# Loading kv in 8 KB rows, and written-out orders for the first and last group of two chained feed-forward layers

## The reference, cut to what matters

```python
# q: 12288 x 128, kv: 384 x 32 x 128
kv_pool = kv.reshape(B, H//4, 4, W//4, 4, C).mean(axis=(2, 4))    # 96 x 8 cells of 4 x 4 pixels
k = v = kv_pool.reshape(B, -1, C) @ w_sr                          # 768 keys
a = softmax(q @ k.T / sqrt(C))                                    # sum gets + 1e-9
x = a @ v
h = x @ w_in1                                                     # 128 -> 2048
x = (max(h, 0) + alpha * min(h, 0)) @ w_out1                      # first layer
h = x @ w_in2                                                     # second layer
out = ((a0 + a1 h + a2 h^2 + a3 h^3) / (1 + |b0||h| + |b1| h^2 + 1e-6)) @ w_out2
```

## Time and profile before

| | |
|---|---|
| median of 3 runs | 1563.15 us (1561.4 to 1563.31) |
| the profiled execution | 1564.52 us; its span in the trace 1562.7 us |
| busy share of the span | TensorE 97%, VectorE 92%, ScalarE 90%, GpSimd 79% |
| load and pooling of kv | up to 36.4 us |
| attention | 36.4 to 322.4 us |
| first layer of group 0 alone | 322.4 to 363.5 us |
| both layers | 363.5 to 1504.6 us |
| second layer of group 23 alone, and the last store | 1504.6 to 1562.7 us |

### The profile page before, as it was taken

How to read it: one execution, slowest core, us unless ns; L and a number is a source line. 1 busy time by engine, 2 the same in 40 slices (tenths; PEclk the granted TensorE clock), 3 DMA queues, 4 the chain that set the end, 5 groups by cost and what they waited for, 6 DMA issues and landing times. The chain is left out here.

```text
span 1562.7 us, 28287 instructions
## 1 busy us (share of the span) xinstructions
PE 1509.7 (97%) x8269; PEld 1242.8 (80%) x8269; DVE 1432.4 (92%) x2257; ACT 1401.7 (90%) x2714; POOL 1237.9 (79%) x1352
## 2 busy tenths in 40 slices
PE   5999999979999999999999999999999999999986
PEld 5899999846788888888888888888888888888865
DVE  4788888727999999999999999999999999999997
ACT  1777777637999999999999999999999999999996
POOL 0444444405999999999999999999999999999998
PEclk9999999999999999999999999999999999999998
DMA  8110110000000000000000000000000000000000
GB/s 244 48 28 22 28 48 21 1 0 1 8 1 8 8 8 8 2 8 8 8 1 8 8 8 8 1 8 8 8 8 1 8 8 8 1 8 8 8 8 8
DMA packets 12330, 24.94 MB, mean 16 GB/s; under 512 B 1536, under 2 KB 1680, under 8 KB 11920
## 3 DMA queue, kind: packets, MB, share of 16 engines
q1 hardware_dynamic: 11424, 22.55, 4.8%
q10 hardware_dynamic: 752, 0.60, 0.1%
HBM read 16.85 MB, written 6.29 MB: 15 GB/s over the span
## 5 line engine op out<-in xcount | busy, mean ns | idle before, releaser
L270 POOL TENSOR_TENSOR cubic<-sq,lin_p 128x512 f32<-128x512 f32 x384 | 495.6, 1291 | 84.3 <-ACT sq L458 59.7
L261 POOL TENSOR_TENSOR rational<-newton,ratio 128x512 f32<-128x512 f32 x336 | 434.0, 1292 | 29.5 <-PE banks L1073 21.2
L1073 PEld LDWEIGHTS banks<-wout,rational 128*128 128x128 f32 x3072 | 399.8, 192 | 44.0 <-issue 11.0
L880 PE MATMUL banks<-x_hi,win_lo 128*128 128x512 f32 x768 | 387.1, 504 | 25.6 <-DVE ratio L747 13.5
L1073 PE MATMUL banks<-wout,rational 128*128 128x128 f32 x3072 | 402.7, 276 | 3.8 <-POOL rational L261 3.8
L882 PE MATMUL banks<-x_hi,win_hi 128*128 128x512 f32 x768 | 303.4, 395 | 0.0
L881 PE MATMUL banks<-x_lo,win_hi 128*128 128x512 f32 x768 | 302.9, 394 | 0.0
L476 ACT ACTIVATE lin_p<-banks,ab_raw 128x512 f32<-128x512 f32 x384 | 298.4, 777 | 1.0 <-PE banks L882 1.0
L730 DVE SCALAR_TENSOR_TENSOR banks<-sq,abs_b,banks 128x512 f32<-128x512 f32 x384 | 286.9, 747 | 2.9 <-ACT banks L468 2.5
L738 DVE SCALAR_TENSOR_TENSOR banks<-banks,ab_raw,cubic 128x512 f32<-128x512 f32 x384 | 288.3, 751 | 0.8 <-POOL cubic L270 0.8
L747 DVE SCALAR_TENSOR_TENSOR ratio<-banks,ab_raw,rcp 128x512 f32<-128x512 f32 x384 | 285.7, 744 | 1.8
(11 more groups left out here) (91 smaller groups left out, 2261.3 us busy)
## 6 DMA issues: line engine op xcount, KB each, us to landing
early<-in_kv_dram SPq DMA_DIRECT2D x24, 256.0 KB, 10.1
out_dram<-y_out SPq DMA_DIRECT2D x24, 256.0 KB, 2.0
neg_part<-in_q_dram SPq DMA_DIRECT2D x22, 256.0 KB, 2.7
early<-in_moe_w_in_dram SPq DMA_DIRECT2D x1, 1024.0 KB, 16.4
wout<-in_moe_w_in_dram SPq DMA_DIRECT2D x1, 1024.0 KB, 5.2
neg_part<-in_q_dram ACTq DMA_DIRECT2D x2, 256.0 KB, 9.3
early<-in_w_sr_dram ACTq DMA_DIRECT2D x1, 64.0 KB, 1.9
wout<-in_moe_w_out_dram SPq DMA_DIRECT2D x2, 0.5 KB, 12.6
```

The source lines that it names most:

```text
L261: nc.gpsimd.tensor_tensor(rational[:, m % 3, :], newton[:, m % 2, :], ratio[:, m % 2, :], ALU.mult).then_inc(s["rat_done"], 1)
L270: nc.gpsimd.tensor_tensor(cubic[:, m % 2, :], sq[:, m % 2, :], lin_p[:, m % 2, :], ALU.mult).then_inc(s["cubic_done"], 1)
L880: nc.tensor.matmul(dst, w[1], x[0], start=start, stop=False)
L1073: last = nc.tensor.matmul(banks[:, ACC2, t * P:(t + 1) * P], rational[:, m % 3, t * P:(t + 1) * P], wout2[:, c, :], start=(c == 0 and t == ...
```

## The change

1. **kv.** A partition now holds one image row (32 pixels) of each third of the image, and a chunk is one half of it: 16 pixels, 8 KB that lie together in memory. Five transfers of 1 MB and two of 512 KB take the place of 24 of 256 KB. A cell is thus spread over four partitions. A chunk has four units of 32 cells; in a unit four pixels lie side by side in a partition. TensorE sums over partitions and pixels at once, with a matrix of 128 x 32 with ones (`row_sums`, made by VectorE from the identity): four matmuls of 32 columns for a unit. For 14 of the 24 units (`BY_DVE_UNITS`) VectorE sums the four pixels first (512 elements to 128), and one matmul is left. The order of the keys changes, for k and v alike.
2. **Coefficients.** Their two broadcasts move from ACT's queue to SP's, behind w_out1, and the Abs of them to behind attention, ahead of the register loads.
3. **End of attention.** The split of w_out1 (`out1_hi`, `out1_lo`) moves into step 24 of attention, and hidden1 of group 0, block 0 into its last step.
4. **First group.** hidden1 has two banks, 0 and 1, in turn while n < 16, and waits for the block before last. The orders of all engines for the periods 0 and 1 are written out.
5. **Last group.** The periods from 24 on are written out for all engines, in an order of their own, and in group 23 VectorE makes five finals (2, 6, 10, 14, 15) in place of two. The loop bodies stay and run for p = 2 to 23.

```diff
 BY_DVE_FINAL, BY_DVE_RELU = (4, 12), (14,)
+LAST_DVE_FINAL = (2, 6, 10, 14, 15)
...
-    kv_rows = kv[0].rearrange("(hh r) (ww x) c -> hh ww r (x c)", r=POOL_SIDE, x=POOL_SIDE)
+    kv_rows = kv[0].rearrange("(k h) (n w) c -> k n h (w c)", h=P, n=2)
+    CELLS = P // POOL_SIDE
+    UNITS = P // CELLS
...
-        DVE_PIXELS, POOLED, VALUES = 2 * POOL_SIDE, (2, 3, 5, 6, 7, 2), (3, 6)
+        BY_DVE_UNITS = ((0, 1, 2), (0, 1), (0, 1), (0, 1, 2), (0, 1), (0, 2))
...
-        H1, ACC1, QV, H2, ACC2 = 0, 2, (3, 4), (5, 6, 1), 7
+        H1, ACC1, QV, H2, ACC2 = (0, 1), 2, (3, 4), (5, 6, 1), 7
...
+        def dve_finals(g):
+            return LAST_DVE_FINAL if g == GROUPS - 1 else BY_DVE_FINAL
...
+        def h1_bank(n):
+            return H1[n % 2 if n < BLOCKS else 0]
...
-            for c in range(CHUNKS):
-                for r in range(POOL_SIDE):
-                    sp.dma_start(kv_in[:, c, r * POOL_SIDE * P:(r + 1) * POOL_SIDE * P],
-                                 kv_rows[c * key_rows:(c + 1) * key_rows, :, r, :]).then_inc(s[f"ld_kv{c}{'aabb'[r]}"], 16)
+            for c in range(CHUNKS - 1):
+                sp.dma_start(kv_in[:, c, :], kv_rows[c // 2, c % 2]).then_inc(s[f"ld_kv{c}"], 16)
+            half = UNITS // 2 * POOL_SIDE * P
+            sp.dma_start(kv_in[:, CHUNKS - 1, 0:half], kv_rows[CHUNKS // 2 - 1, 1, :, 0:half]).then_inc(s[f"ld_kv{CHUNKS - 1}"], 16)
+            sp.dma_start(kv_in[:, CHUNKS - 1, half:], kv_rows[CHUNKS // 2 - 1, 1, :, half:]).then_inc(s["ld_kv_rest"], 16)
             sp.dma_start(raw_in[0], w_in1).then_inc(s["ld_in1"], 16)
             sp.dma_start(wout1[:], w_out1.rearrange("(b p) c -> p b c", p=P)).then_inc(s["ld_out1"], 16)
+            sp.dma_start(ab_raw[:, 0:4], coef_p.partition_broadcast(P)).then_inc(s["ld_ab"], 16)
+            sp.dma_start(ab_raw[:, 4:6], coef_q.partition_broadcast(P)).then_inc(s["ld_ab"], 16)
...
+                if g == GROUPS:
+                    out1_hi()
...
+            act.wait_ge(s["ld_ab"], 32)
+            nc.scalar.activation(abs_b[:], ab_raw[:, 4:6], ACT.Abs).then_inc(s["absb_col_done"], 1)
+            act.wait_ge(s["absb_col_done"], 1)
             scale_b0, scale_a3 = act.alloc_register("scale_b0"), act.alloc_register("scale_a3")
...
+                for u in BY_DVE_UNITS[c]:
+                    if c == CHUNKS - 1 and u >= UNITS // 2:
+                        dve.wait_ge(s["ld_kv_rest"], 16)
+                    pixels = kv_in[:, c, u * POOL_SIDE * P:(u + 1) * POOL_SIDE * P]
+                    nc.vector.tensor_reduce(pooled[:, c, u, :], pixels.rearrange("p (x n) -> p n x", x=POOL_SIDE),
+                                            AX.X, ALU.add).then_inc(s["pooled_done"], 1)
...
+                for u in by_pe:
+                    if c == CHUNKS - 1 and u >= UNITS // 2:
+                        pe.wait_ge(s["ld_kv_rest"], 16)
+                    for x in range(POOL_SIDE):
+                        at = (u * POOL_SIDE + x) * P
+                        nc.tensor.matmul(banks[:, POOLED[c], u * CELLS:(u + 1) * CELLS], kv_in[:, c, at:at + P], row_sums,
+                                         start=(u == by_pe[0] and x == 0), stop=False, skip_group_check=True)
+                for n, u in enumerate(BY_DVE_UNITS[c]):
+                    pe.wait_ge(s["pooled_done"], made_before + n + 1)
+                    last = nc.tensor.matmul(banks[:, POOLED[c], u * CELLS:(u + 1) * CELLS], pooled[:, c, u, :], row_sums,
+                                            start=False, stop=(n == len(BY_DVE_UNITS[c]) - 1), skip_group_check=True)
...
+                if g == STEPS - 1:
+                    hidden1(0, 0)
...
+                    n = g * BLOCKS + c
+                    if n >= 2:
+                        negative_ready(pe, n - 2 if n < BLOCKS else n - 1)
+                    hidden(h1_bank(n), win1_hi, win1_lo, c, g).then_inc(s["h1_ready"], 1)
...
-            for p in range(GROUPS + 3):
+            hidden1(0, 1)
+            linear(0)
+            hidden1(0, 2)
+            out1(0, 0)
+            hidden1(0, 3)
+            hidden1(0, 4)
+            out1(0, 1)
+            out1(0, 2)
...
+            for p in range(2, GROUPS):
```

More of the change, by code:

```diff
@@ L448, in negative @@
                     after(act, s["m1_done"], n - 3)
-                    kept = neg_hi if c in SPLIT else neg_part
-                    nc.scalar.activation(kept[:, c // 2 % 2, :], banks[:, H1, :], ACT.Relu).then_inc(s["neg_done"], 1)
+                    part = neg_hi if c in SPLIT else neg_part
+                    nc.scalar.activation(part[:, c // 2 % 2, :], banks[:, h1_bank(n), :], ACT.Relu).then_inc(s["neg_done"], 1)
             def square(g, c):
@@ L889, in pooled_transpose @@
             def pooled_transpose(c):
-                dst = banks[:, POOLED[c], 0:P]
+                by_pe = [u for u in range(UNITS) if u not in BY_DVE_UNITS[c]]
+                made_before = sum(len(units) for units in BY_DVE_UNITS[:c])
                 if c == 4:
@@ L1142, in _ @@
                 out1(p - 1, 15)
+            hidden2(GROUPS - 3, 15)
+            hidden1(GROUPS - 1, 1)
+            out2(GROUPS - 3, 10)
+            out2(GROUPS - 3, 11)
+            out2(GROUPS - 3, 12)
+            hidden2(GROUPS - 2, 0)
+            linear(GROUPS - 1)
+            hidden1(GROUPS - 1, 2)
+            hidden2(GROUPS - 2, 1)
+            out1(GROUPS - 1, 0)
+            hidden1(GROUPS - 1, 3)
+            out1(GROUPS - 1, 1)
+            hidden2(GROUPS - 2, 2)
+            out2(GROUPS - 3, 13)
@@ new lines, in _ @@
+            out2(GROUPS - 3, 14)
+            hidden2(GROUPS - 2, 3)
+            hidden1(GROUPS - 1, 4)
+            out2(GROUPS - 3, 15)
+            hidden1(GROUPS - 1, 5)
+            out1(GROUPS - 1, 2)
+            hidden2(GROUPS - 2, 4)
+            out1(GROUPS - 1, 3)
+            out1(GROUPS - 1, 4)
+            hidden1(GROUPS - 1, 6)
+            hidden2(GROUPS - 2, 5)
+            out2(GROUPS - 2, 0)
+            hidden1(GROUPS - 1, 7)
+            out2(GROUPS - 2, 1)
+            hidden2(GROUPS - 2, 6)
@@ new lines, in _ @@
+            out1(GROUPS - 1, 5)
+            hidden1(GROUPS - 1, 8)
+            hidden2(GROUPS - 2, 7)
+            out1(GROUPS - 1, 6)
+            hidden1(GROUPS - 1, 9)
+            out2(GROUPS - 2, 2)
+            hidden2(GROUPS - 2, 8)
+            out2(GROUPS - 2, 3)
+            out2(GROUPS - 2, 4)
+            out1(GROUPS - 1, 7)
+            hidden1(GROUPS - 1, 10)
+            hidden2(GROUPS - 2, 9)
+            out1(GROUPS - 1, 8)
+            hidden1(GROUPS - 1, 11)
+            out1(GROUPS - 1, 9)
@@ new lines, in _ @@
+            hidden2(GROUPS - 2, 10)
+            out2(GROUPS - 2, 5)
+            hidden2(GROUPS - 2, 11)
+            out2(GROUPS - 2, 6)
+            hidden1(GROUPS - 1, 12)
+            out1(GROUPS - 1, 10)
+            hidden1(GROUPS - 1, 13)
+            hidden2(GROUPS - 2, 12)
+            out2(GROUPS - 2, 7)
+            hidden1(GROUPS - 1, 14)
+            out1(GROUPS - 1, 11)
+            hidden2(GROUPS - 2, 13)
+            hidden1(GROUPS - 1, 15)
+            out1(GROUPS - 1, 12)
+            out1(GROUPS - 1, 13)
@@ new lines, in _ @@
+            out2(GROUPS - 2, 8)
+            hidden2(GROUPS - 2, 14)
+            out2(GROUPS - 2, 9)
+            hidden2(GROUPS - 2, 15)
+            out1(GROUPS - 1, 14)
+            out1(GROUPS - 1, 15)
+            out2(GROUPS - 2, 10)
+            out2(GROUPS - 2, 11)
+            hidden2(GROUPS - 1, 0)
+            hidden2(GROUPS - 1, 1)
+            out2(GROUPS - 2, 12)
+            hidden2(GROUPS - 1, 2)
+            hidden2(GROUPS - 1, 3)
+            out2(GROUPS - 2, 13)
+            out2(GROUPS - 2, 14)
```

607 lines of the change are left out of this document (553 added, 54 removed).

## The result

The kernel with the change takes **1551.55 us** (median of 6 runs, 1550.99 to 1552.39), against 1562.93 before (1559.87 to 1563.31). The ratio is 0.9931 [0.9921, 0.9941], so it is 11.4 us faster, less than half of the 24.3 us forecast, and 1551.55 lies above the range of 1533 to 1548. The profiled span went from 1562.7 to 1550.4 us.

The account below looks back on a forecast made before the run. Stages have their own limits: kv transfer, TensorE in attention, three engines in the pipeline, so only earlier block starts or a shorter end count. 10.6 + 12.4 + 1.3 = 24.3 us, giving 1538.9 against the median; range 1533 to 1548.

Parts of the forecast that it names:

- TensorE's part of the pooling: kv pooling before attention: 54 small matmuls take at most the old step, 13.6 us in 17, covered by the stream.
- rival 2: Start: 32-column matmuls get half clock, pooling ends at about 34, front worth nothing; gain 13.7, 1549.5 us; chance 0.07.
- The front: kv load and pooling up to the first scores: first scores at 25.8 us, 10.6 us earlier; ends 3.2 and 12.4.
- the end: Last second layer: new orders and finals gain 2.2 - 1.8 + 0.9 = 1.3 us; ends -0.9 and 2.8.
- the middle: First layer of group 0, after attention: 14.5 us less 2.1 of stalls, 12.4 us gained; ends 7.2 and 14.5.
- the pipeline: Layers between the lone first and last ones: moves as a block, 1141 us as before, within 1.
- rival 4: Clock held low far into attention, kernel slower than before: 1576 us at 75 us of half speed; chance 0.02.
- a granted clock under 1 before 60 us: Start of the kernel: one of the signs written down that would show the forecast wrong.
- The stream: kv load in 8 KB rows: 392 GB/s in place of 278, last piece at 21.2 us.
- The broadcasts as the cause of the 98 GB/s: Load from 4 to 7 us: the slow stretch comes from two coefficient broadcasts and goes when they leave ACT's queue.
- VectorE's unit: Pooling on VectorE: a unit of 512 elements costs 0.95 us, 14 units 13.3 us.
- the 2.1 us of stalls charged: First layer of group 0: 1.2 us for ScalarE's Abs and register loads, 0.4 chain waits, 0.5 clock.

Follow-up runs that it names:

- e1: The changed kernel with each of the 54 pooling matmuls 128 moving columns wide (ones between zeros) in place of 32: 1540.14 us.
- e2: The changed kernel, pooling still narrow, with 12 unused 128-column identity matmuls on TensorE ahead of the first kv piece: 1551.55 us.
- e3: The changed kernel with the old kv load and old pooling put back, the coefficient broadcasts staying on SP behind w_out1: 1546.63 us.
- e11: e1 with the Abs of the coefficients and the register loads moved into step 8 of attention: 1539.7 us.

## Why the prediction was wrong, point by point

**The failed step is TensorE's part of the pooling**: "TensorE's 54 small matmuls against 54 before take at most the old step". The shape had changed, and I took the old duration as an upper bound, since a narrower matmul has less to do. In place of 13.6 us the 108 records took 24.6 (80 of 392 ns and 28 of 401; before, 108 took 16.1, with the slow first sixteen), because TensorE's clock was at the lower level; e1 and e2 show that it is the clock, and that it stands at the upper level with the same matmuls 128 columns wide. From 7.03 to 34.9 us TensorE is the bound, and nothing of the faster stream arrives. That is rival 2 in its mechanism: it had the pooling end "at about 34" (seen: 34.9), and gave 1549.5. That its number comes within about 2 us is partly luck. The front (-0.8), attention (-1.0) and the end (-2.1) gave less than it had, and the middle (+1.8) and the pipeline (+0.7) more.

**Why rival 2 had 0.07.** I read "1.00 from 2 to 7 us with TensorE all but idle" as a full clock at rest, and let it outweigh the rule of the Trainium skill. e2 and the changed kernel show the same step of 3.46 us, once beside 0.50 and once beside 1.00, so the column's 1.00 at the start of a trace was no measurement. The start was slow before, too, as the rule would have it: 3.65 us for the sixteen records at 11.13, in the stretch that rival 4 cites for its 1.00. A hint was in the rows shown: the old matmuls took 275 ns, but 580 at most. For the same reason my sign of being wrong, "a granted clock under 1 before 60 us", could not show in this trace. Durations of one shape tell the clock where the column can't.

**The stream**: right in kind, and faster than taken (413 to 423 GB/s against 392). The 358 GB/s per core of the Trainium skill ("DMA: Bandwidth & Descriptors", Where 436 GB/s comes from), by which I had worked out a second sum, doesn't hold here, over 10 us and more. The Trainium skill's other page on it ("HBM Reference", Specifications (TRN2)) says that a core streaming alone gets about 425 GB/s; with one core running, that was the rule to weigh, and these windows agree with it.

**The broadcasts as the cause of the 98 GB/s**: right (e3). With them away the first scores came 4.35 us earlier, about 2 of them from the stretch itself. It had been inside the term of 10.6, so its size had never been stated by itself.

**VectorE's unit**: 1.02 us in place of 0.95. **First scores at 25.8**: 26.14 once TensorE has its clock. With e1 the forecast's sum comes back: 24.3 forecast, 24.4 by the spans (1562.7 - 1538.3), 22.9 by the medians. That it fits so well is luck in part: the middle gave 1.8 more than forecast, the end 1.5 less.

**Middle**: right in mechanism, 14.2 against 12.4 and inside its ends. Of the 2.1 us of stalls charged, the clock (0.5) did not fall at all. ScalarE's head cost 1.06 (e11) against 1.2; the other 1.1 us are TensorE's own work and the small waits of the chain, counted too high.

**Pipeline**: 1140.4 to 1141.2 us in all profiles; the block moved as a whole.

**End**: forecast 1.3, seen nothing that can be told from 0. The tail behind the last quotient did become shorter (0.9 forecast, 0.9 to 1.7 seen in nine profiles of ten), but how much of it is the final's and how much the clock's is open. Wrong was the removal of 2.2 us of VectorE's waits as "GpSimd's". GpSimd is busy 46.1 in place of 49.3 us (first fence and the earlier trace rows), and of VectorE's waits only 1.2 us had ended with it. In the changed kernel these are gone (in e1 one of 0.7 stands), and 1.7 us that end with TensorE and 1.9 with ScalarE stand in their place, where it had been 0.8 and none. What brought them, the order or the finals themselves, no run takes apart.

## What to carry to other kernels

When a change narrows matmuls or opens pauses between them, look at the duration of one shape before and after, ahead of the clock column, and try the same kernel with the width kept: here zeros in the moving data, four times the work on paper, gave back 11 us. Price each part of a combined change by itself: here a second bank carried the gain, moving two small broadcasts gave 4 us, and the headline part was a loss until its matmuls were wide.

## What was not expected of the hardware

- Matmuls of 32 and of 128 moving columns with a fresh 128x128 fp32 weight load each take the same at full clock: 1.21 and 1.16 us for eight records.
- TensorE busy 10.00 of 10 us, about three quarters of its records of the 32-column form, was granted 0.50 (e2), and so for over 20 us; in e1 the 128-column form, busy 9.67 of 10, ran at 0.12 us a record.
- With two broadcasts of a few bytes for each partition beside the first rows of kv, the 16 DMA engines moved 98 GB/s for 3 us, busy 0.40 of the time; without them it was 281 at 1.01 (e3). Behind w_out1 they cost nothing that these traces show.
